# Recurrent attention and two routed layers on one core: earlier tables, one-instruction placing, gates placed in the layer's head

## The reference

```python
for t in range(S):                               # attention
    cur = einsum('bhd,bhe->bhde', u * k[t], v[t])
    y[t] = einsum('bhd,bhde->bhe', r[t], state + cur)
    state = w[..., None] * state + einsum('bhd,bhe->bhde', k[t], v[t])
x = y as [3072, 384]
# layer 1: rows with x @ w_skip <= 0 pass through; layer 2 has no skip and no "x +"
logits = x @ w_gate                              # [rows, 8]
e_idx = argmax(logits); gate_w = softmax(logits)[e_idx]
for e in range(8):
    h = maximum(x[e_idx == e] @ w1[e], 0)        # 384 -> 1024
    y[e_idx == e] = gate_w * (h @ w2[e])         # 1024 -> 384
out = x + y  (layer 1)      out = y  (layer 2)
```

## Time and profile before

| | |
|---|---|
| median of 3 runs | 594.66 us (594.61 to 594.92) |
| the profiled execution, its own time | 589.84 us |
| its span from first to last instruction | 588.1 us |
| PE busy | 539.8 us (92%) |
| DVE, ACT, POOL busy | 387.9, 251.9, 249.9 us |
| attention | 0 to 134 us |
| route 1, layer 1 | 134 to 154, 154 to 300 us |
| route 2, layer 2 | 300 to 342, 342 to 588 us |

### The profile page before, as it was taken

One profiled execution on the slowest core, in us unless ns is written; L12 is line 12 of the kernel. 1 busy time (PEld: TensorE's weight loads), 2 busy tenths in 40 slices (PEclk: granted clock), 3 DMA queues, 4 the chain that ended last, 5 costly groups with the idle time before them and its releaser, 6 DMA issues. The chain is left out here.

```text
span 588.1 us, 16050 instructions
## 1 busy us (share of the span) xinstructions
PE 539.8 (92%) x5550; PEld 512.8 (87%) x5551; DVE 387.9 (66%) x839; ACT 251.9 (43%) x704; POOL 249.9 (42%) x348
## 2 busy tenths in 40 slices
PE   3999999988799999999857879999999999999992
PEld 3899998978699999999855769999999999999992
DVE  5888888867688878888613927463747464647330
ACT  0233333334077667776413017362736352626220
POOL 5887778742244444454410043232534323324331
PEclk9999999997899999999969989999999999999997
DMA  9798888876187777776378014544444534111100
GB/s 140 121 188 165 161 161 162 169 254 224 43 312 223 209 230 250 244 236 212 60 245 304 0 54 115 185 157 147 139 165 153 162 140 147 50 46 43 39 15 26
DMA packets 114127, 89.58 MB, mean 152 GB/s; under 512 B 80672, under 2 KB 104931, under 8 KB 114080
## 3 DMA queue, kind: packets, MB, share of 16 engines
q1 hardware_dynamic: 106304, 74.16, 45.1%
q0 software_dynamic: 7776, 14.82, 9.1%
HBM read 80.44 MB, written 13.27 MB: 159 GB/s over the span
## 5 line engine op out<-in xcount | busy, mean ns | idle before, releaser
L822 DVE TENSOR_TENSOR w_lo<-w_raw,w_hi 128x384 fp32r<-128x384 f32 (+1 forms) x224 | 130.2, 608 | 4.7 <-ACT w_hi L817 3.1
L1092 PE MATMUL e_ps_h<-e_x_hi,w_hi 128*128 128x192 f32 (+3 forms) x384 | 119.6, 311 | 3.2 <-DVE e_x_lo L1210 2.9
L817 ACT CAST w_hi<-w_raw 128x384 fp32r<-128x384 f32 (+1 forms) x224 | 119.9, 566 | 3.8 <-issue 3.5
L1094 PE MATMUL e_ps_h<-e_x_hi,w_lo 128*128 128x192 f32 (+3 forms) x384 | 119.6, 311 | 0.0
L1093 PE MATMUL e_ps_h<-e_x_lo,w_hi 128*128 128x192 f32 (+3 forms) x384 | 119.5, 311 | 0.0
L1250 DVE SCALAR_TENSOR_TENSOR e_h_lo<-e_ps_h,e_h_hi 128x128 fp32r<-128x128 f32 (+1 forms) x192 | 70.5, 396 | 44.5 <-ACT e_h_hi L1179 40.1
L1092 PE MATMUL e_ps_y<-w_hi,e_h_hi 128*128 128x384 f32 x272 | 95.5, 351 | 0.0
L1094 PE MATMUL e_ps_y<-w_hi,e_h_lo 128*128 128x384 f32 x272 | 91.5, 336 | 0.0
L1093 PE MATMUL e_ps_y<-w_lo,e_h_hi 128*128 128x384 f32 x272 | 91.1, 335 | 0.0
L1092 PEld LDWEIGHTS e_ps_h<-e_x_hi,w_hi 128*128 128x128 f32 x384 | 72.9, 190 | 5.4 <-DVE e_x_lo L1210 3.4
L1094 PEld LDWEIGHTS e_ps_h<-e_x_hi,w_lo 128*128 128x128 f32 x384 | 72.9, 190 | 1.2
(11 more groups left out here) (168 smaller groups left out, 922.4 us busy)
## 6 DMA issues: line engine op xcount, KB each, us to landing
w_raw<-in_moe_w_dram SPq DMA_DIRECT2D x32, 1536.0 KB, 7.3
r_in<-in_r_dram SPq DMA_DIRECT2D x24, 192.0 KB, 3.2
k_in<-in_k_dram SPq DMA_DIRECT2D x24, 192.0 KB, 3.9
v_in<-in_v_dram SPq DMA_DIRECT2D x24, 192.0 KB, 4.0
x_rows<-rows SPq DMA_DIRECT2D x24, 192.0 KB, 3.5
w_lo<-x_rows SPq DMA_DIRECT2D x6, 768.0 KB, 6.6
x_in<-x_rows,e_ent_in POOLq DMA_INDIRECT x33, 3.1
out_dram<-y_rows,e_ent_out POOLq DMA_INDIRECT x19
```

Of the source, the lines that this page charges most:

```text
L817: act.copy(self._of(self.hi1[par], self.hi2[par], n), self._of(self.raw1[par], self.raw2[par], n)).then_inc(self.hi_done[par], 1)
L822: eng.tensor_tensor(self._of(self.lo1[par], self.lo2[par], n), self._of(self.raw1[par], self.raw2[par], n), self._of(self.hi1[par], self.h ...
L1092: pe.matmul(o, s_hi, m_hi, start=(k == 0), stop=False)
L1094: return pe.matmul(o, s_lo, m_hi, start=False, stop=(k == last))
```

## The change

Five edits.

- **Early tables.** w goes straight into `w_pow`, and w and u are loaded through ACT's queue, so SP begins with r. r and k are counted apart from v (`rk_loaded`, `v_loaded`). POOL zeroes only the padding columns. `shrink` is built on POOL by doubling, beside DVE's `grow`, without a reciprocal. `shrink_up` is made behind the first `rk`, and PE transposes it behind the scores of step 0.
- **Placing.** The place is split in float arithmetic. `col_hot` (compare with the column, times the row number) and `row_hot` are made by one DVE `tensor_scalar` each per tile, 48 in all. PE's matrix for the table is 38 (45) columns wide instead of 76 (90).
- **Gates in the layer's head.** The gates get their own 24 DVE instructions (`gate_hot`) and their own 24 matmuls at the start of `moe`, in place of one of three turns of `stay_warm`. `result` waits for them.
- **x loads of two tiles.** Each DMA of `load_rows` becomes two.
- The last wait on the scatters moves from POOL to SP, `e_iota` is made first, and the entries lose their second word.

```diff
 attention
-            sp.wait_ge(dve_zeroed, 2)
-            for j in range(2):
-                sp.dma_start(w_col[PAD * j:PAD * j + D, :], w..., ...).then_inc(small, 16)
-            sp.dma_start(u_row[:], ...).then_inc(small, 16)
...
-                pool.memset(r_in[n][:], 0.0).then_inc(zeroed, 1)
+                pool.memset(r_in[n][:, :, D:PAD], 0.0).then_inc(zeroed, 1)
...
+            pool.memset(shrink[:, :, HALF - 1:HALF], 1.0).then_inc(shrunk, 1)
+            for n in range(6):
+                m = 2 ** n
+                pool.wait_ge(shrunk, n + 1)
+                pool.wait_ge(tables, POWERS[n])
+                pool.tensor_tensor(shrink[:, :, HALF - 2 * m:HALF - m], shrink[:, :, HALF - m:HALF], w_pow[:, n, :].unsqueeze(2).to_broadcast([P, NP, m]), ALU.mult).then_inc(shrunk, 1)
+            pool.wait_ge(shrunk, 7)
+            pool.wait_ge(tables, LOW)
+            pool.tensor_tensor(shrink[:, :, HALF:P], shrink[:, :, 0:HALF], grow[:, :, 0:1].to_broadcast([P, NP, HALF]), ALU.mult).then_inc(shrunk, 1)
...
+            act.dma_start(u_row[:], u.rearrange("h d -> (h d)").partition_broadcast(P)).then_inc(u_loaded, 16)
...
-            link(dve.reciprocal(shrink[:, :, 0:P // 2], grow[:, :, 1:P // 2 + 1]))
-            link(dve.tensor_tensor(shrink[:, :, P // 2:P], ...))
-            link(dve.tensor_tensor(shrink_up[:], shrink[:], ...))
+            dve.wait_ge(shrunk, 8)
             rk(0, 0)
+            dve.tensor_tensor(shrink_up[:], shrink[:], ...).then_inc(tables, 1)
 load_rows
-    eng.dma_start(dst, ...[g]).then_inc(x_loaded[g], 16)
+    for n in range(2):
+        eng.dma_start(dst[:, half * n:half * n + half, :], src[:, half * n:half * n + half, :]).then_inc(x_loaded[2 * g + n], 16)
 route
-                dve.tensor_tensor(col_is[:], row_iota..., col_i..., ALU.is_equal)
-                dve.tensor_tensor(col_hot[:, i, 1, :], col_is[:], entry[:, i, 1]..., ALU.mult)
-                dve.tensor_tensor(col_hot[:, i, 0, :], col_is[:], entry[:, i, 0]..., ALU.mult)
-                for place in range(PLACES // 2 * n, PLACES // 2 * (n + 1)):
-                    rows_hot(dve, place)
+            for place in range(PLACES):
+                for i in range(GP * place, GP * place + GP):
+                    dve.tensor_scalar(col_hot[:, i, :], col_iota, col[:, i:i + 1], ids[:, i:i + 1], ALU.is_equal, ALU.mult)
+                    ins = dve.tensor_scalar(row_hot[:, i, :], row_iota[:], row[:, i:i + 1], None, ALU.is_equal)
+                ins.then_inc(hots_ready, 1)
 moe, PE
-            stay_warm(pe, ident, ps_y[0][:, 0:P], 3)
+            for i in range(TILES):
+                pe.wait_ge(gates_hot, i + 1)
+                ins = pe.matmul(ps_y[1][:, 0:USED], row_hot[:, i, :].bitcast(F32), gate_hot[:, i, :], start=(i == 0), stop=(i == TILES - 1))
+            ins.then_inc(gates_placed, 1)
+            stay_warm(pe, ident, ps_y[0][:, 0:P], WARM)      # WARM = 2
 moe, DVE
             start_spans(dve)
+            for i in range(TILES):
+                dve.tensor_scalar(gate_hot[:, i, :], col_iota[:, 0:USED], col[:, i:i + 1], gate[:, i:i + 1], ALU.is_equal, ALU.mult).then_inc(gates_hot, 1)
+            dve.wait_ge(gates_placed, 1)
+            dve.tensor_copy(gates[:, 0:USED], ps_y[1][:, 0:USED]).then_inc(gates_out, 1)
```

More of the change, by code:

```diff
@@ L397, in step @@
                 ins.then_inc(scored, 1)
+                if isinstance(i, int) and i == 0:
+                    pe.wait_ge(tables, TABLE_STEPS + 1)
+                    for p in range(NP):
+                        ins = pe.transpose(ps_x[:, P * p:P * p + P], shrink_up[:, p, :], ident[:])
+                    ins.then_inc(tab_ps, 1)
                 if sub == 1 and not (isinstance(c, int) and c == 0):
@@ L431, in load_rows, with route @@
     dst = x_in[g % len(x_in)]
-    eng.dma_start(dst, x_rows.rearrange("(b c p) d -> c p b d", b=dst.shape[1], p=P)[g]).then_inc(x_loaded[g], 16)
-def route(nc, m, W, x_rows, ident, w_g, lg, NCOL, table, starts, order, stored, x_in, x_loaded, fresh_rows):
+    src = x_rows.rearrange("(b c p) d -> c p b d", b=dst.shape[1], p=P)[g]
+    half = dst.shape[1] // 2
+    for n in range(2):
+        eng.dma_start(dst[:, half * n:half * n + half, :], src[:, half * n:half * n + half, :]).then_inc(x_loaded[2 * g + n], 16)
+def route(nc, m, W, x_rows, ident, w_g, lg, NCOL, table, starts, order, stored, x_in, x_loaded, row_tiles, hots):
     tag = f"m{m + 1}"
@@ L591, in _ @@
             if not TURN:
-                for row in fresh_rows:
-                    pool.memset(row[:], 0.0).then_inc(made, 1)
-                pool.memset(table[:, NCOL:table.shape[1], :], NOWHERE).then_inc(made, 1)
+                for row_tile in fresh_rows:
+                    pool.memset(row_tile[:], 0.0).then_inc(made, 1)
+                pool.memset(table[:, NCOL:table.shape[1]], NOWHERE).then_inc(made, 1)
                 pool.wait_ge(made, 8 + len(fresh_rows))
@@ L762, in _ @@
             dve.wait_ge(placed, PLACES)
[L763 to L764 removed]
+            dve.tensor_scalar(table[:, 0:NCOL], ps_placed, float(NOWHERE), None, ALU.add)
 class Weights:
@@ L828, in wait_split, with moe @@
         eng.wait_ge(self.lo_done[k][par], (self.N1, self.N - self.N1)[k] * (pair + 1))
-def moe(nc, m, W, rows, out_rows, ident, USED, table, starts, x_in, y_rows, load_next):
+def moe(nc, m, W, rows, out_rows, ident, USED, table, starts, x_in, y_rows, load_next, h_parts, hots):
     tag = f"e{m}"
@@ L859, in moe @@
         x_lo = sb("x_lo", [P, DC, XW], F32R)
-        h_hi = sb("h_hi", [P, FC, XW], F32R)
-        h_lo = sb("h_lo", [P, FC, HALF + XW], F32R)
+        h_hi, h_lo = h_parts
+        row_hot, gate, row, col, row_iota, col_iota = hots
+        TILES = gate.shape[1]
+        gate_hot = sb("gate_hot", [P, TILES, USED])
+        WARM = 2
+        gates = sb("gates", [P, USED + 4])
         top_at = XW if m else 0
```

174 lines of the change are left out of this document (83 added, 91 removed).

## The result

| | before | after |
|---|---|---|
| median | 594.63 us (594.0 to 594.92, 4 runs) | 613.74 us (613.15 to 614.83, 4 runs) |
| ratio, 95% interval | | 1.0325 [1.0307, 1.0343] |
| profiled execution, its span | 589.84, 588.1 | 613.15, 611.4 |
| mean granted clock over the span | 0.971 | 0.942 |

Slower by 19.1 us in the medians and by 23.3 between the two profiled executions; 6.1 were forecast. The two traces are read side by side at the starts of the same stages. Differences are after less before, in us.

What follows compares the result with a forecast made beforehand. Bound: PE's unchanged body work plus what lies ahead of each layer's first product. Terms -1.15 + 4.8 - 0.95 + 0.7 + 4.6 - 1.9 = +6.1 us on 594.66 gave 600.8 us, range 594.0 to 605.0.

Steps and rivals of the forecast that it cites:

- Heads: Start of each layer: gate passes at 0.112 us warm, 14 pieces cold then 54 warm; +4.8 us layer 1, +4.6 layer 2.
- Routes: Placing in both routes: 24 one-hot pairs on DVE in 5.45 us, PE then last; -0.95 us route 1, -1.9 route 2.
- plain-rate rival: Routes: DVE one-hots at the plain rate take 7.5 us, giving +0.1 and -0.7; total 603.0 us, chance 0.23.
- x loads: Ahead of layer 2's PE start: eight half-size issues on SP instead of four; +0.7 us, ends 0 and +2.5.
- Attention: Attention's start: earlier tables and loads, most of 4.6 us given back behind POOL; -1.15 us, ends -4.6 and 0.
- Other edits: Last wait on SP, smaller entries: beside PE's work or changing places at the end; costed at nothing.
- The late ACT copy: Rival, route 2: ACT's 4.8 us stand before a copy disappears, 3.9 us of it on the path; 596.9 us, chance 0.09.
- Moving columns: Rival, heads and routes: a 38-column pass costs half a 76-column one, 0.057 us warm; total 593.6 us, chance 0.13.
- The clock not falling: Rival, heads: PE's clock stays up, 14 pieces at 0.112 us, -1.6 us in each head; 597.6 us, chance 0.07.

Runs made afterwards that it cites:

- a_first: Kernel after with 24 warm-up turns of the identity ahead of the gate passes and none behind them: 612.34 us, ratio to before 1.0295.
- a_wide: Kernel after with each head's 48 gate passes reading their 38 or 45 columns three times over: 604.89 us, ratio to before 1.0153.
- e_dve: Kernel after with 30 extra DVE instructions of several kinds and widths in layer 1's head, to time each: 613.54 us, one run.
- a_xwhole: Kernel after with before's whole x loads, four tiles a load: 612.07 us, ratio to before 1.0299.
- b_end: Kernel before with the last scatter wait moved from GpSimd to SP's end: 592.49 us, ratio to before 0.9969.
- b_attn: Kernel before with the new attention alone (early tables, r and k loaded ahead of v): 592.58 us, ratio to before 0.999.
- a_all: Kernel after with gate and placing passes reading columns two or three times, one-hots by wide instructions, and whole x loads: 592.96 us, ratio to before 0.9986.
- a_tt: Kernel after with the routes' one-hots made by wide DVE instructions over several tiles: 609.3 us, ratio to before 1.0262.
- b_best: Kernel before with the new attention and the last scatter wait at SP's end: 591.97 us, ratio to before 0.9973.

## Why the prediction was wrong

The direction was right, the size a third of what came. By its terms:

- **Heads, +4.8 and +4.6: the step that failed.** Measured +9.9 and +9.6. "14 cold in 3.2 us, 54 warm": that the clock rises some 3 us after PE starts was read from transposes of 128 columns and carried over to passes of 38. With those PEclk stayed at 0.50 through all 48 passes and, in layer 1, the 16 transposes behind them. The price of a warm pass (0.112) was nearly right (0.117 in a_first). Where the clock does rise as I took it to, in a_wide, the first product comes 11.74 and 14.22 us after PE's start; my sum was 11.9 and 13.6. So nearly the whole error of the term is the clock, shown by a_wide and a_first.
- **Routes, -0.95 and -1.9.** Measured +2.4 and +1.95. The one-hots took 9.76 us; my range was 3.4 to 7.5 and I took the middle. I had read 0.19 us for 38 columns as columns plus an overlap of 0.085; e_dve shows 0.07 fixed and 0.06 for each pointer, and after has two of them in half of its instructions. The range was drawn from rows without a pointer that mattered. Even the plain-rate rival was too cheap. The copy that made me take the middle did not show what I read from it: no `tensor_tensor` ran beside POOL's fills, the first starts at 7.21, when they have ended. That single-source instructions are faster per column was right all the same (e_dve).
- **x loads, +0.7** with ends 0 and +2.5: measured +2.54 in the trace, the upper end. Each issue has its price (a_xwhole).
- **Attention, -1.15**: -0.99 at route 1's first one-hot, a hit that may be luck, as two executions of the old attention differ by 2.0 us there. `k_end` starts at 15.15 (15.46 forecast), before 16.61; that most of the earlier start is given back behind POOL was right.
- **Other edits, 0**: the wait on SP gives 2.0 to 2.3 (b_end).
- **The late ACT copy** The earlier trace rows did not go, it moved: DVE stands 4.98 us at 330.50 with no engine named, and the stage takes 1.4 us more. I had no term for it. b_attn shows the same 1.4 with the new attention alone.
- **Rivals.** Moving columns: no, 0.117 for 38. The clock not falling: the opposite. Plain rate: nearest in cause for the routes, still short. None of them had the clock held down by the work itself.

Forecast against the profile: +6.1; the terms as measured: -1.0 +2.4 +9.9 -1.0 +2.5 +1.4 +1.95 +9.6 -0.2 -2.3 = +23.3.

**Open:** layer 1's body (first product to last scatter) was 1.0 us shorter in after: 135.02 us against 135.98, and 135.0 to 135.2 against 136.2 to 136.3 in a_all, a_xwhole and a_tt against b_end, b_attn and b_best. It is in neither the attention's edit nor the moved wait; no run separates it further.

## To carry over

Before placing small matmuls where the PE must be fast afterwards, look at the granted clock: here passes of 38 and 45 columns kept PE busy and still left it at half speed. Reading the same columns three times costs a pass nearly nothing at 1.00 (0.119 us against 0.117) and was worth 9 us. Count a per-tile DVE instruction by its fixed part and its pointers before its columns, and compare with one wide instruction over several tiles. When runs of one kernel scatter, look at where the clock falls: a few turns in PE's waits can be worth more than a clever edit.

## Not expected of the hardware

- Passes of 38 columns, back to back with PE fully busy: PEclk 0.50 for their 10.3 us and for the transposes behind them (156 to 170); and from 1.00 to 0.50 near the end of 5.6 us of them (a_first). With 114 columns: 1.00 some 4 us after PE's start.
- The clock can be lost over gaps of 0.3 to 1.1 us between small pieces of work (b_end, 349 to 354). The products then run at 0.50 up to 358.5, which costs about 2 us.
- With the last wait on scatters at SP's end the program closes 6.5 us after the last scatter's issue, with it on GpSimd 8.5 to 8.8.
- DVE: 0.07 us an instruction, 0.06 a pointer, 0.52 and 1.05 ns a column (e_dve).
